# A float32 attention stage rewritten ahead of two expert stages, on one core of Trainium2

## The chip, the cores and the metric

The kernel runs on one core of one Trainium2 chip. The metric is the device time of one execution in microseconds (us). Engines are named as in the profile: PE is TensorE (its weight loads are PEld), DVE is VectorE, ACT is ScalarE, POOL is GpSimd, SP is SyncE, whose queue issues most DMAs here.

## What is computed

Three stages follow each other on 1536 tokens (2 batches of 768), all in float32.

```python
# attention: 2 x 8 heads, 768 positions, head size 64, n_sink = 4, window = 128
scores = scale * q @ k.T
keep = is_sink | ((rel >= 0) & (rel < window))
a = softmax(where(keep, scores, -1e9));  x = a @ v        # -> [1536, 512]
# SoLU block: 512 -> 1024 -> 512
h = x @ w_in;  solu = h * softmax(h);  x = (layernorm(solu) * g_ln) @ w_out
# eight dense experts, 512 -> 1024 -> 512, weighted by a Sinkhorn-normalised gate P
P = exp(x @ w_gate - max)
for _ in range(8): P /= rowsum(P); P /= colsum(P); P *= N / E
out = sum_e P[:, e] * (relu(x @ w1[e]) @ w2[e])
```

## The kernel before

Every engine has its own program, written out by hand, and semaphores between them. The engines take their instructions in order, so the order in the code is the order of the work.

**Products by splitting.** A float32 number is held as two float32r parts, `hi` (rounded) and `lo` (the rest). `three` multiplies with three matmuls (hi by hi, hi by lo, lo by hi) of 128x512, lines L495 to L497. Where a product is taken in float32 instead, the profile shows two MATMULs for one of the code.

**Attention.** The 16 heads go in eight pairs (`PAIRS`); a pair has 12 steps (`STEPS`), one head's six query tiles of 128 and then the other's. For tile t the scores are 128 x 128, 128 x 256 or, from t=2 on, 128 x 260: two blocks of keys and the four sinks.

- Loads: SP brings q and k of a head, each twice over 128 partitions, and v, and one segment of `w_in` and `w_out` beside each pair.
- Splits of q and k: POOL (`split_qk`, L324 to L335) rounds q (768 columns), subtracts on 64 partitions, rounds k and subtracts, once per head; for the first pair ACT and DVE help.
- Scores, PE L407 to L412: `q_stack` holds q's hi and lo one above the other, so two matmuls (k_hi, k_lo) make the product, and two of 4 columns the sinks. Three PSUM banks.
- `mask_max`, DVE L906: adds the mask, scales and takes the row's largest value, from PSUM to `probs` in SBUF. `exp_tile`, ACT L753: exponential and row sum.
- `invert`, DVE: L914 adds 1e-9 to six sums, L917 inverts them, L921 multiplies the sink columns. `normalise`, DVE L929: 128 x 256 from SBUF to SBUF, one instruction a tile.
- `turn`, PE L436: 22 transposes a pair of 128x128 blocks, in six groups through two banks; `turn_sinks` L443. `copy_pT`: five groups are copied from PSUM to SBUF by ACT (L759), one by DVE.
- `pv`, PE L474: float32 products of v and the turned probabilities, one head in output partitions 0 to 63 and the other in 64 to 127; `pv_sinks` L484, one product of 8 rows and 512 columns.
- `round_x` on ACT and `rest_x` on DVE (L957) split the result. `round_segments` on ACT and `rest_w_in`, `rest_w_out` on DVE (L943, L948) split the weight segments.

The pairs run in a pipeline: while pair i+1 has its scores, pair i is turned and multiplied (`body`, a hardware loop over pairs 1 to 6 on each engine).

**SoLU block.** `h1_half(T, n)` is 12 matmuls; the first four halves are set among the last pair's turns. DVE, ACT and POOL do softmax and layernorm; then transposes, `wout`, and the second split of x.

**Experts.** 16 units of half an expert. `hidden(u, g)` makes 12 groups of 12 matmuls, `expert_out(u, T)` 12 tiles of 12. POOL splits the weights: `split_unit(j)` rounds 2048 columns (L373) and subtracts (L375). Unit j=0 goes to `w_first`, j=1 to `w_unit[2:4]`, j=2 to `w_unit[0:2]`. The gate is computed by DVE between the groups of `hidden(0)`: `divide_rows` and `divide_cols` (L1125 to L1139), eight times each, with PE summing the columns by a matmul (L703) that waits for the rows. After the last one DVE copies the gate and frees PSUM banks: `y_free` starts at 2, which lets PE do two tiles of `expert_out`, and L1186 adds two.

Of the kernel before, what the change touches and what calls it, by code (L numbers as in the profile page):

```python
# [24 lines left out]
F32 = mybir.dt.float32  # L25
F32R = mybir.dt.float32r
# [33 lines left out]
def solu_moe(nc: bass.Bass, n_sink, window, qT, kT, v, w_in, w_out, g_ln, w_gate, w_exp, out):  # L60
# [5 lines left out]
    with ExitStack() as ctx:  # L66
# [34 lines left out]
        q_raw = sb("q_raw", [P, 2, SEQ], F32, in_a)  # L101
        k_raw = sb("k_raw", [P, 2, SEQ], F32, in_a)
        q_stack = sb("q_stack", [P, 2, SEQ], F32R, in_a)
        k_hi = sb("k_hi", [P, 2, SEQ], F32R, in_a)
        k_lo = sb("k_lo", [P, 2, SEQ], F32R, in_a)
        v_sb = sb("v_sb", [P, 2, QT * DH], F32, in_a)
        v_sink = sb("v_sink", [2 * NS, P], F32, in_a)
        probs = sb("probs", [P, STEPS, PW], F32, in_a)
# [4 lines left out]
        mask0 = sb("mask0", [P, P], F32, in_a)  # L113
        mask1 = sb("mask1", [P, 2 * P], F32, in_a)
        mask2 = sb("mask2", [P, PW], F32, in_a)
        a_stat = sb("a_stat", [P, 4, STEPS], F32, in_a)
# [21 lines left out]
        q_loaded = [sem(f"q_loaded{h}") for h in range(2)]  # L138
        k_loaded = [sem(f"k_loaded{h}") for h in range(2)]
        v_loaded = [sem(f"v_loaded{h}") for h in range(2)]  # L140
        vs_loaded = sem("vs_loaded")
# [9 lines left out]
        first_rounded, qk_rounded = sem("first_rounded"), sem("qk_rounded")  # L151
        q_split, k_split = sem("q_split"), sem("k_split")
        scores_full, scores_read = sem("scores_full"), sem("scores_read")
        exp_done = sem("exp_done")
        norm_link = sem("norm_link")
# [4 lines left out]
        va_used = sem("va_used")  # L160
        x_full, x_hi_out, x_out = sem("x_full"), sem("x_hi_out"), sem("x_out")
        seg_hi, seg_done = sem("seg_hi"), sem("seg_done")
# [24 lines left out]
        S_BANKS, ST_BANK, T_BANK, X_BANK = 3, 3, 4, 6  # L187
        X0 = 2 * P
# [4 lines left out]
        def p_block(h, n):  # L193

            t = (n + 1) // 2
            at = P if (n % 2 == 0 and t > 0) else 0
            return probs[:, QT * h + t, at:at + P]

        def t_group(m):

            h, g = divmod(m, 3)
            return h, 4 * g, min(4 * g + 4, NBLK)

        PT_ON_ACT = (0, 1, 3, 4, 5)
        PT_ON_DVE = (2,)
# [25 lines left out]
        def _(sp):  # L231
            def load_q(p, h):
                sp.dma_start(q_raw[:, h, :], qT[p, h]).then_inc(q_loaded[h], 16)

            def load_k(p, h):
                sp.dma_start(k_raw[:, h, :], kT[p, h]).then_inc(k_loaded[h], 16)
# [6 lines left out]
            for h in range(2):  # L243
                load_q(0, h)
                load_k(0, h)
            for h in range(2):
                sp.dma_start(v_sb[:, h, :], v[0, h]).then_inc(v_loaded[h], 16)
            sp.wait_ge(consts, 4)
            for h in range(2):
                sp.dma_start(v_sink[h * NS:(h + 1) * NS, h * DH:(h + 1) * DH],  # L250
                             v[0, h, 0:NS, 0:DH]).then_inc(vs_loaded, 16)
            sp.dma_start(g_col[:, :], g_ln).then_inc(small_loaded, 16)
            sp.dma_start(wg_raw[:, :, :], w_gate).then_inc(small_loaded, 16)
            load_segments(0)

            def load_next(i):

                for h in range(2):
                    sp.wait_ge(q_split, 2 * i + (h + 1))
                    load_q(i + 1, h)  # L260
                    sp.wait_ge(k_split, 2 * i + (h + 1))
                    load_k(i + 1, h)

            def load_beside(i):

                sp.wait_ge(seg_done, 2 * i)
                load_segments(i)
                sp.wait_ge(va_used, i)
                sp.dma_start(v_sb[:, 0, :], v[i, 0]).then_inc(v_loaded[0], 16)

            load_next(0)
            with sp.Fori(1, PAIRS - 1) as i:
                load_next(i)
                load_beside(i)
            load_beside(PAIRS - 1)

            sp.wait_ge(seg_done, 2 * FC)
# [11 lines left out]
        def _(pool):  # L289
# [30 lines left out]
            def split_qk(p, h):  # L320

                pool.wait_ge(q_loaded[h], 16 * p + 16)
                pool.sem_inc(pool_passed, 1)
                pool.tensor_scalar(q_stack[:, h, :], q_raw[:, h, :], 1.0, 0.0,  # L324
                                   ALU.mult, ALU.add).then_inc(qk_rounded, 1)
                pool.wait_ge(qk_rounded, 4 * p + (2 * h + 1 - 4))
                pool.tensor_tensor(q_stack[64:128, h, :], q_raw[64:128, h, :],
                                   q_stack[64:128, h, :].bitcast(F32), ALU.subtract).then_inc(q_split, 1)
                pool.wait_ge(q_split, 2 * p + (h + 1))
                pool.wait_ge(k_loaded[h], 16 * p + 16)  # L330
                pool.sem_inc(pool_passed, 1)
                pool.tensor_scalar(k_hi[:, h, :], k_raw[:, h, :], 1.0, 0.0,
                                   ALU.mult, ALU.add).then_inc(qk_rounded, 1)
                pool.wait_ge(qk_rounded, 4 * p + (2 * h + 2 - 4))
                pool.tensor_tensor(k_lo[:, h, :], k_raw[:, h, :], k_hi[:, h, :].bitcast(F32),  # L335
                                   ALU.subtract).then_inc(k_split, 1)


            pool.wait_ge(masks, 4)
            pool.wait_ge(q_split, 1)  # L340
            pool.wait_ge(k_split, 1)
            pool.wait_ge(first_rounded, 3)
            pool.tensor_tensor(q_stack[64:128, 1, :], q_raw[64:128, 1, :],
                               q_stack[64:128, 1, :].bitcast(F32), ALU.subtract).then_inc(q_split, 1)
            pool.wait_ge(q_split, 2)
            pool.wait_ge(first_rounded, 4)
            pool.tensor_tensor(k_lo[:, 1, :], k_raw[:, 1, :], k_hi[:, 1, :].bitcast(F32),
                               ALU.subtract).then_inc(k_split, 1)
            with pool.Fori(1, PAIRS) as p:
                for h in range(2):  # L350

                    pool.wait_ge(scores_full, STEPS * p + (QT * h - QT))
                    split_qk(p, h)


# [38 lines left out]
        def _(pe):  # L394
            def scores(p, k):

                h, t = divmod(k, QT)
                if t == 0:
                    pe.wait_ge(q_split, 2 * p + (h + 1))
                    pe.wait_ge(k_split, 2 * p + (h + 1))  # L400
                if not (isinstance(p, int) and STEPS * p + k < S_BANKS):
                    pe.wait_ge(scores_read, STEPS * p + (k - S_BANKS + 1))
                o = bank(k % S_BANKS)
                q = q_stack[:, h, t * P:(t + 1) * P]
                lo = max(t - 1, 0) * P
                hi = (t + 1) * P
                pe.matmul(o[:, 0:hi - lo], q, k_hi[:, h, lo:hi], start=True, stop=False)  # L407
                last = pe.matmul(o[:, 0:hi - lo], q, k_lo[:, h, lo:hi], start=False, stop=True)  # L408
                if t >= 2:
                    pe.matmul(o[:, 2 * P:PW], q, k_hi[:, h, 0:NS], start=False, stop=False,  # L410
                              skip_group_check=True)
                    last = pe.matmul(o[:, 2 * P:PW], q, k_lo[:, h, 0:NS], start=False, stop=True,  # L412
                                     skip_group_check=True)
                last.then_inc(scores_full, 1)

            def turn(p, m):

                h, n0, n1 = t_group(m)
                if m % 3 == 0:
                    pe.wait_ge(probs_ready, 2 * p + (h + 1))  # L420

                if m >= 2:
                    free = m - 2
                    pair = 0
                else:
                    free = m + 4
                    pair = -1
                if free in PT_ON_ACT:
                    n = len(PT_ON_ACT)
                    pe.wait_ge(pT_act, n * p + (n + n * pair + PT_ON_ACT.index(free) + 1))  # L430
                else:
                    n = len(PT_ON_DVE)
                    pe.wait_ge(pT_dve, n * p + (n + n * pair + PT_ON_DVE.index(free) + 1))
                o = bank(T_BANK + m % 2)
                for n in range(n0, n1):
                    last = pe.transpose(o[:, (n - n0) * P:(n - n0 + 1) * P], p_block(h, n), ident[:, :])  # L436
                last.then_inc(pT_full, 1)

            def turn_sinks(p):

                pe.wait_ge(sinkT_out, p + 1)
                for t in range(2, QT):
                    last = pe.transpose(bank(ST_BANK)[0:2 * NS, (t - 2) * P:(t - 1) * P],  # L443
                                        sinks[:, t - 2, :], ident[:, :])
# [784 lines left out]
```

## Time and profile before

| | |
|---|---|
| three runs | 1359.62, 1362.14, 1365.0 us; median 1362.14 |
| the profiled execution | 1365.01 us, its span 1363.2 us |
| mean granted TensorE clock | 0.984 |
| PE busy | 1322.8 us, 97% of the span |
| DVE, ACT, POOL busy | 498.5 us (37%), 259.1 (19%), 319.5 (23%) |
| DMA | 56.94 MB, mean 42 GB/s |

The busy shares are means over three very different stages: attention until about 148 us, the SoLU block until about 308 us, then the gate and the experts. Each has to be read by itself. Matmuls are pipelined and their ends modelled, so the distance from one start to the next says more than a duration.

### The profile page before, as it was taken

The numbers are of one execution on the slowest core, as the hardware profiler recorded it, in microseconds if no ns is written. First come the engines' busy times: TensorE is split into PE (matmuls) and PEld (weight loads), VectorE is DVE, ScalarE is ACT, GpSimd is POOL, SyncE is SP. The second block draws the span as 40 slices with busy tenths as digits, with TensorE's granted clock in tenths as the row PEclk, the third lists the DMA queues.
The fourth block names the chain that finished last, engine by engine and source line by source line (L and its number), as shares of the span: only waits on it lengthen the run. The fifth ranks groups of instructions, "written<-read, shape, count | busy, mean of one in ns | idle before, by whom it ended". The sixth has DMA issues, their size and how long they took to land.

```text
span 1363.2 us, 16251 instructions
## 1 busy us (share of the span) xinstructions
PE 1322.8 (97%) x6103; PEld 1088.8 (80%) x6103; DVE 498.5 (37%) x964; ACT 259.1 (19%) x555; POOL 319.5 (23%) x179
## 2 busy tenths in 40 slices
PE   5888999998999999999999999999999999999999
PEld 5666788876888888888888888888888888888887
DVE  6888553526422222222222222222222222222222
ACT  5655543421010102020101010111101010101020
POOL 6555021332011112222211111111111111111110
PEclk9888999999999999999999999999999999999999
DMA  5442200001000000000011100000000000000002
GB/s 167 147 146 95 64 0 1 1 31 62 0 31 31 31 31 31 31 31 31 31 33 44 46 31 31 31 31 31 31 31 31 31 31 31 31 31 31 31 0 93
DMA packets 15988, 56.94 MB, mean 42 GB/s; under 512 B 2144, under 2 KB 4192, under 8 KB 11872
## 3 DMA queue, kind: packets, MB, share of 16 engines
q1 hardware_dynamic: 14848, 55.28, 11.8%
q10 hardware_dynamic: 1120, 1.39, 0.3%
q8 instruction: 13, 0.21, 0.1%
q14 instruction: 7, 0.06, 0.0%
HBM read 53.51 MB, written 3.15 MB: 42 GB/s over the span
## 4 chain that ended last, share of the span: by engine, by line
PE 91%; DVE 5%; issue 2%; ACT 1%; DVEq 0%; ACTq 0%
PE ps L495 28%; PE ps L497 28%; PE ps L496 28%; PE ps L436 2%; DVE probs L929 1%; DVE probs L906 1%; PE ps L407 1%; PE ps L474 1%; PE ps L576 1%; PE ps L408 1%; PE ps L484 1%; PE ps L443 0%; DVE acc L1038 0%; ACT acc L812 0%; PE ps L412 0%
## 5 line engine op out<-in xcount | busy, mean ns | idle before, releaser
L495 PE MATMUL ps<-w_unit,h_hi 128*128 128x512 f32 x768 | 298.9, 389 | 0.0
L497 PE MATMUL ps<-w_unit,h_lo 128*128 128x512 f32 x768 | 298.8, 389 | 0.0
L496 PE MATMUL ps<-w_unit,h_hi 128*128 128x512 f32 x768 | 298.8, 389 | 0.0
L884 ACT ACTIVATE h_hi<-ps 128x512 fp32r<-128x512 f32 x192 | 114.9, 598 | 908.2 <-PE ps L497 908.2
L495 PE MATMUL ps<-x_hi,w_unit 128*128 128x512 f32 x720 | 280.1, 389 | 0.0
L496 PE MATMUL ps<-x_lo,w_unit 128*128 128x512 f32 x720 | 280.1, 389 | 0.0
L497 PE MATMUL ps<-x_hi,w_unit 128*128 128x512 f32 x720 | 280.1, 389 | 0.0
L1182 DVE SCALAR_TENSOR_TENSOR acc<-ps,gate_now,acc 128x512 f32<-128x512 f32 x192 | 144.2, 751 | 355.5 <-PE ps L497 355.5
L1107 DVE SCALAR_TENSOR_TENSOR h_lo<-ps,h_hi 128x512 fp32r<-128x512 f32 x192 | 132.7, 691 | 385.2 <-ACT h_hi L884 385.2
L373 POOL TENSOR_SCALAR w_unit<-w_raw 128x2048 fp32r<-128x2048 f32 x31 | 59.5, 1919 | 813.1 <-PE ps L497 808.0
L495 PEld LDWEIGHTS ps<-w_unit,h_hi 128*128 128x128 f32 x768 | 144.1, 188 | 30.1
L497 PEld LDWEIGHTS ps<-w_unit,h_lo 128*128 128x128 f32 x768 | 144.1, 188 | 29.9
L496 PEld LDWEIGHTS ps<-w_unit,h_hi 128*128 128x128 f32 x768 | 144.1, 188 | 29.9
L495 PEld LDWEIGHTS ps<-x_hi,w_unit 128*128 128x128 f32 x720 | 135.1, 188 | 28.2
L497 PEld LDWEIGHTS ps<-x_hi,w_unit 128*128 128x128 f32 x720 | 135.1, 188 | 28.0
L496 PEld LDWEIGHTS ps<-x_lo,w_unit 128*128 128x128 f32 x720 | 135.1, 188 | 28.0
L375 POOL TENSOR_TENSOR w_unit<-w_raw,w_unit 128x2048 fp32r<-128x2048 f32 x31 | 142.8, 4605 | 2.6
L407 PE MATMUL ps<-k_hi,q_stack 128*128 128x256 f32 (+1 forms) x96 | 42.2, 439 | 19.5 <-DVE a_stat L906 12.4
L753 ACT ACTIVATE probs<-probs,a_stat 128x260 f32<-128x260 f32 (+1 forms) x96 | 46.7, 487 | 55.2 <-DVE a_stat L906 54.9
L436 PE MATMUL ps<-ident,probs 128*128 128x128 f32 x176 | 36.4, 339 | 11.6 <-DVE probs L929 9.3
L407 PEld LDWEIGHTS ps<-k_hi,q_stack 128*128 128x128 f32 x96 | 24.2, 253 | 27.2 <-DVE a_stat L906 16.9
L929 DVE TENSOR_SCALAR probs<-probs,a_stat 128x256 f32<-128x256 f32 (+1 forms) x96 | 44.9, 484 | 0.0
(129 smaller groups left out, 1120.7 us busy)
## 6 DMA issues: line engine op xcount, KB each, us to landing
w_raw<-w_exp SPq DMA_DIRECT2D x32, 1024.0 KB, 4.8
q_raw<-qT SPq DMA_DIRECT2D x16, 384.0 KB, 4.3
k_raw<-kT SPq DMA_DIRECT2D x16, 384.0 KB, 3.9
out<-acc SPq DMA_DIRECT2D x12, 256.0 KB, 2.0
w_raw<-w_in SPq DMA_DIRECT2D x8, 256.0 KB, 2.6
w_raw<-w_out SPq DMA_DIRECT2D x8, 256.0 KB, 2.9
v_sb<-v SPq DMA_DIRECT2D x9, 192.0 KB, 2.4
v_sb<-v ACTq DMA_DIRECT2D x7, 192.0 KB, 2.9
```

Source lines behind the costliest of these rows:

```text
L373: pool.tensor_scalar(hi, w_raw[:, :], 1.0, 0.0, ALU.mult, ALU.add).then_inc(unit_rounded, 1)
L375: pool.tensor_tensor(lo, w_raw[:, :], hi.bitcast(F32), ALU.subtract).then_inc(unit_split, 1)
L407: pe.matmul(o[:, 0:hi - lo], q, k_hi[:, h, lo:hi], start=True, stop=False)
L436: last = pe.transpose(o[:, (n - n0) * P:(n - n0 + 1) * P], p_block(h, n), ident[:, :])
L495: pe.matmul(o, ws[0], xs[0], start=first, stop=False)
L496: pe.matmul(o, ws[0], xs[1], start=False, stop=False)
L497: return pe.matmul(o, ws[1], xs[0], start=False, stop=last)
L753: act.activation(probs[:, k, 0:w], probs[:, k, 0:w], ACT.Exp, bias=a_stat[:, A_NMAX, k:k + 1], scale=-1.0, accum_out=a_stat[:, A_SUM, k:k ...
L884: act.activation(h_hi[:, g, :], bank(g % 4), ACT.Relu).then_inc(h_hi_out, 1)
L929: last = dve.tensor_scalar(probs[:, k, 0:w], probs[:, k, 0:w], a_stat[:, A_INV, k:k + 1], None, ALU.mult)
L1107: dve.scalar_tensor_tensor(out=h_lo[:, g, :], in0=bank(g % 4), scalar=0.0, in1=h_hi[:, g, :].bitcast(F32), op0=ALU.max, op1=ALU.subtract). ...
L1182: dve.scalar_tensor_tensor(out=acc[:, T, :], in0=bank(4 + T % 4), scalar=gate_now[:, T:T + 1], in1=acc[:, T, :], op0=ALU.mult, op1=ALU.add ...
```

## The change

- **Scores** are float32 products, one matmul a tile, with q and k as loaded. The two heads of a pair lie on partitions 0 to 63 and 64 to 127 (`q_sb`, `k_sb`), and step t does both heads one after the other in the queue, into two of four banks. `split_qk` goes. `k_sb` holds for each tile its 256 keys and the four sinks next to them, so SP issues four DMAs a head for q and k (one with 16-byte pieces). q, k, v are double-buffered by pair.
- **Inverse sums** stay on DVE, now for four tiles at a time (three times a pair), and `normalise` moves to POOL, four tiles at a time (`BATCHES`).
- **Turns** go in three batches of both heads (3, 4 and 4 blocks), and the sinks' turn takes its place in the same two banks (`SINK_USE`), after the second use and its pair. ACT copies uses 0, 2, 4, 5, DVE copies 1, 3, 6. `turn` of batch 0 is at step t=4 of its own pair, those of batches 1 and 2 at t=0 and t=2 of the next.
- **Weight segments**: rounding and subtracting both on POOL (`round_segments`, `rest_w_in`, `rest_w_out`).
- The loops over pairs are written out.
- **Experts**: `split_unit(1)` follows `split_unit(0)` and writes the free half of `w_first`; `split_unit(2)` waits for the eighth row division (`rows_done`).

```diff
+            def load_qk(p, h):
+                rows_h = slice(64 * h, 64 * h + 64)
+                k_ph = kT[p, h][0:DH]
+                sp.dma_start(q_sb[rows_h, p % 2, :], qT[p, h][0:DH]).then_inc(qk_loaded[p % 2], 16)
...
             for h in range(2):
-                load_q(0, h)
-                load_k(0, h)
+                load_qk(0, h)
             for h in range(2):
-                sp.dma_start(v_sb[:, h, :], v[0, h]).then_inc(v_loaded[h], 16)
+                load_qk(1, h)
             sp.wait_ge(consts, 4)
             for h in range(2):
+                load_v(0, h)
+            load_segments(0)
...
+            for p in range(1, PAIRS):
+                if p >= 2:
+                    sp.wait_ge(scores_full, STEPS * (p - 1))
+                    for h in range(2):
+                        load_qk(p, h)
+                sp.wait_ge(in_done, p)
+                sp.wait_ge(out_done, p)
+                load_segments(p)
+                if p >= 2:
+                    sp.wait_ge(x_full, p - 1)
+                    for h in range(2):
+                        load_v(p, h)
...
+            def normalise(p, b):
+
+                pool.wait_ge(inv_ready, BATCHES * p + b + 1)
+                for k in range(4 * b, 4 * b + 4):
+                    w = min(k // 2 + 1, 2) * P
+                    last = pool.tensor_scalar(tile_probs(p, k)[:, 0:w], tile_probs(p, k)[:, 0:w],
+                                              a_stat[:, A_INV, k:k + 1], None, ALU.mult)
+                last.then_inc(probs_ready, 1)
...
+            round_segments(0)
+            for p in range(PAIRS):
+                normalise(p, 0)
+                rest_w_in(p)
+                normalise(p, 1)
+                rest_w_out(p)
+                normalise(p, 2)
+                if p + 1 < PAIRS:
+                    round_segments(p + 1)
...
             split_unit(0, w_first[:, 0, 0:UW], w_first[:, 1, 0:UW])
+            split_unit(1, w_first[:, 0, UW:2 * UW], w_first[:, 1, UW:2 * UW])
             pool.wait_ge(lnT_full, NB * FC)
             pool.memset(acc[:, :, :], 0.0).then_inc(acc_zero, 1)
             pool.wait_ge(o_full, o_index(NB - 1, DC - 1) + 1)
-            split_unit(1, w_unit[:, 2, :], w_unit[:, 3, :])
+            pool.wait_ge(rows_done, SINKHORN)
             split_unit(2, w_unit[:, 0, :], w_unit[:, 1, :])
...
+                for h in range(2):
+                    k = 2 * t + h
+                    n = STEPS * p + k
+                    if n >= S_BANKS:
+                        pe.wait_ge(scores_read, n - S_BANKS + 1)
+                    rows_h = slice(64 * h, 64 * h + 64)
+                    w = width(t)
+                    pe.matmul(bank(k % S_BANKS)[:, 0:w], q_sb[rows_h, p % 2, t * P:(t + 1) * P],
+                              k_sb[rows_h, p % 2, k_at(t), 0:w], start=True, stop=True).then_inc(scores_full, 1)
...
+            def back(p, t):
+
+                if t == 0 and p > 0:
+                    turn(p - 1, 1)
+                if t == 1 and p > 0:
+                    pv(p - 1, 1)
+                if t == 2 and p > 0:
+                    turn_sinks(p - 1)
+                    turn(p - 1, 2)
+                if t == 3 and p > 0:
+                    pv(p - 1, 2)
+                    pv_sinks(p - 1)
+                if t == 4:
+                    turn(p, 0)
+                if t == 5:
+                    pv(p, 0)
...
+            for p in range(PAIRS):
+                for t in range(QT):
+                    scores(p, t)
+                    back(p, t)
             h1_half(0, 0)
+            back(PAIRS, 0)
             h1_half(0, 1)
+            back(PAIRS, 1)
             h1_half(1, 0)
+            back(PAIRS, 2)
             h1_half(1, 1)
+            back(PAIRS, 3)
...
+            for p in range(PAIRS):
+                for t in range(QT):
+                    if t == 4 and p > 0:
+                        round_x(p - 1)
+                    for h in range(2):
+                        exp_tile(p, 2 * t + h)
+                    back(p, t)
```

ACT's `back` copies batch 1 of head 0 at t=0, the turned sinks and batch 2 at t=2, batch 0 at t=4. DVE's `back` is this:

```diff
+                if t == 0 and p > 0:
+                    invert(p - 1, 2)
+                    copy_pT(p - 1, 1, 1)
+                if t == 2:
+                    invert(p, 0)
+                    if p > 0:
+                        copy_pT(p - 1, 2, 1)
+                if t == 4:
+                    invert(p, 1)
+                    if p > 0:
+                        rest_x(p - 1)
+                    copy_pT(p, 0, 1)
```

## Rows read from the trace of the kernel before

**Rows 1.** Windows: busy time of each engine, granted clock, DMA share, GB/s.

```profile
core 0: us, PE busy (x) PEld busy (x) DVE busy (x) ACT busy (x) POOL busy (x), PEclk, DMA share, GB/s
29.50:137.05 107.55, 89.75 (x577) 71.40 (x577) 93.02 (x281) 64.45 (x202) 62.92 (x47) 0.83 0.38 124
30.00:34.00 4.00, 4.00 (x21) 3.65 (x22) 1.95 (x5) 2.44 (x7) 3.70 (x3) 1.00 0.02 4
148.15:166.09 17.94, 17.94 (x98) 13.11 (x99) 8.09 (x19) 6.25 (x12) 1.95 (x3) 1.00 0.21 72
...
322.00:324.00 2.00, 2.00 (x7) 1.61 (x7) 1.56 (x8) 0.00 (x0) 0.00 (x0) 0.50 0.71 147
...
345.00:1363.20 1018.20, 1014.99 (x4478) 839.93 (x4476) 285.04 (x404) 108.30 (x181) 189.32 (x58) 1.00 0.09 32
```

**Rows 2.** Groups by line and shape, DVE, 29.5 to 137.05 us: count, busy, mean.

```profile
L929 DVE TENSOR_SCALAR probs<-probs,a_stat 128x256 f32<-128x256 f32 x60 | 31.4, 524 | 0.0
L906 DVE CUSTOM_DVE_ANT_0 probs<-ps,mask 128x260 f32<-128x260 f32 x49 | 20.3, 414 | 0.9 <-PE ps L412 0.8
L921 DVE TENSOR_TENSOR sinks<-probs,a_stat 128x16 f32<-128x16 f32 x12 | 13.7, 1138 | 0.4
L914 DVE TENSOR_SCALAR a_stat<-a_stat 128x6 f32<-128x6 f32 x12 | 9.5, 792 | 0.1
...
L957 DVE TENSOR_TENSOR x_lo<-ps,x_hi 128x512 f32 x5 | 3.4, 675 | 0.0
```

**Rows 3.** Order of time, DVE and POOL: start, duration, instruction.

```profile
68.46 0.17 DVE L914 TENSOR_SCALAR a_stat<-a_stat 128x6 f32<-128x6 f32 x1
...
77.28 0.83 POOL L332 TENSOR_SCALAR k_hi<-k_raw 128x768 fp32r<-128x768 f32 x1 [0.22 <-POOL q_stack L327]
...
78.05 2.10 DVE L929 TENSOR_SCALAR probs<-probs,a_stat 128x128 f32<-128x128 f32 x2
...
78.19 1.81 POOL L335 TENSOR_TENSOR k_lo<-k_raw,k_hi 128x768 fp32r<-128x768 f32 x1
```

**Rows 4.** The chain of waits, one piece: start, duration, instructions.

```profile
29.50 1.11 PE ps L436 x4
```

**Rows 5.** Order of time, PE, 72 to 79 us.

```profile
72.33 1.08 PE L474 MATMUL ps<-pT,v_sb 128*64 128x256 f32 x8 [0.36 <-ACT pT L759]
...
76.59 1.12 PE L484 MATMUL ps<-sinkT,v_sink 8*128 8x512 f32 x2
77.64 0.66 PE L436 MATMUL ps<-ident,probs 128*128 128x128 f32 x4
78.05 0.36 PE L407 MATMUL ps<-k_hi,q_stack 128*128 128x256 f32 x1
...
78.51 0.36 PE L407 MATMUL ps<-k_hi,q_stack 128*128 128x256 f32 x1
```

**Rows 6.** Order of time in the gate: POOL, DVE, PE.

```profile
316.99 4.49 POOL L375 TENSOR_TENSOR w_unit<-w_raw,w_unit 128x2048 fp32r<-128x2048 f32 x1
...
317.23 4.37 DVE L1128 TENSOR_TENSOR gate<-gate,rows 128x96 f32<-128x96 f32 x1
...
321.66 0.74 PE L703 MATMUL ps<-gate,ones 128*128 128x96 f32 x2 [4.51 <-DVE gate L1128]
```

**Rows 7.** Groups by line and shape, ACT, 0 to 210 us.

```profile
L753 ACT ACTIVATE probs<-probs,a_stat 128x260 f32<-128x260 f32 x64 | 32.2, 504 | 5.9 <-DVE a_stat L906 5.7
```

**Rows 8.** Order of time at the start: SP's queue and PE.

```profile
5.71 0.43 SPq L241 DMA_DIRECT2D w_raw<-w_out  x1
...
7.11 0.45 PE L407 MATMUL ps<-k_hi,q_stack 128*128 128x128 f32 x1 [7.11 <-DVE k_lo L975]
```

**Rows 9.** The page's DMA issues: count, KB, us from issue to landing.

```profile
w_raw<-w_out SPq DMA_DIRECT2D x8, 256.0 KB, 2.9
```

**Rows 10.** Order of time at the gate's end: DVE and PE.

```profile
347.11 0.26 DVE L1128 TENSOR_TENSOR gate<-gate,rows 128x96 f32<-128x96 f32 x1
...
347.84 0.49 PE L495 MATMUL ps<-w_unit,h_hi 128*128 128x512 f32 x1
...
350.33 0.17 DVE L1186 COPY rows<-rows 128x12 f32<-128x12 f32 x1
```

More of the change, by code:

```diff
@@ L339, in _ @@
[L339 to L348, printed above, removed]
@@ L394, in _, with scores @@
         def _(pe):
-            def scores(p, k):
-                h, t = divmod(k, QT)
+            def scores(p, t):
                 if t == 0:
[L399 to L436, printed above, removed]
-                last.then_inc(pT_full, 1)
@@ new lines, in bank_free, with turn @@
+            def bank_free(p, use):
+                before = T_USES * p + use - 2
+                if before >= 0:
+                    done, n = copied(*divmod(before, T_USES))
+                    pe.wait_ge(done, n)
+            def turn(p, b):
+                pe.wait_ge(probs_ready, BATCHES * p + b + 1)
+                for h in range(2):
+                    use = t_use(b, h)
+                    bank_free(p, use)
+                    for n in range(T_FIRST[b], T_END[b]):
+                        at = (n - T_FIRST[b]) * P
+                        last = pe.transpose(t_bank(p, use)[:, at:at + P], p_block(p, h, n), ident[:, :])
+                    last.then_inc(pT_full, 1)
@@ L723, in _ @@
                               stop=True).then_inc(top_all, 1)
-            with pe.Fori(0, UNITS - 1) as u:
+            second = (w_unit[:, 2, :], w_unit[:, 3, :])
+            for T in range(NT):
+                expert_out(0, T, (w_first[:, 0, UW:2 * UW], w_first[:, 1, UW:2 * UW]))
+            for g in range(GROUPS):
+                hidden(1, g, (w_unit[:, 0, :], w_unit[:, 1, :]))
+            with pe.Fori(1, UNITS - 1) as u:
                 for T in range(NT):
-                    expert_out(u, T)
+                    expert_out(u, T, second)
                 for g in range(GROUPS):
@@ L788, in _ @@
-            act.activation(wg[:, :, 0:EXPERTS], wg_raw[:, :, :], ACT.Copy).then_inc(wg_ready, 1)
-            def body(i, before):
-                for k in range(STEPS):
-                    back(i, k)
-                    exp_tile(i + 1, k)
-                    if k == 2 and before:
-                        round_x(i - 1)
-                        load_v(i, 1)
-                        load_sinks(i)
-                    if k == QT - 1:
-                        round_segments(i)
-            body(0, False)
@@ L803, in _, with back @@
-            with act.Fori(1, PAIRS - 1) as i:
-                body(i, True)
+                act.activation(x_hi[:, p * SEQ:(p + 1) * SEQ], x_psum(0, QT), ACT.Copy).then_inc(x_hi_out, 1)
+            def back(p, t):
+                if t == 0 and p > 0:
+                    copy_pT(p - 1, 1, 0)
+                if t == 2 and p > 0:
+                    copy_sinkT(p - 1)
+                    copy_pT(p - 1, 2, 0)
+                if t == 4:
+                    copy_pT(p, 0, 0)
+            for p in range(PAIRS):
+                for t in range(QT):
+                    if t == 4 and p > 0:
+                        round_x(p - 1)
+                    for h in range(2):
+                        exp_tile(p, 2 * t + h)
+                    back(p, t)
+                if p == 0:
+                    act.wait_ge(small_loaded, 32)
+                    act.activation(wg[:, :, 0:EXPERTS], wg_raw[:, :, :], ACT.Copy).then_inc(wg_ready, 1)
@@ L993, in behind @@
-            def behind(p, k):
-                if k < QT:
-                    spread(p, 1, k)
-            for k in range(STEPS):
-                front(0, k)
-            dve.wait_ge(wg_ready, 1)
-            dve.tensor_tensor(wg[:, :, EXPERTS:2 * EXPERTS], wg_raw[:, :, :],
-                              wg[:, :, 0:EXPERTS].bitcast(F32), ALU.subtract).then_inc(wg_ready, 1)
-            def body(i, before):
-                for k in range(STEPS):
-                    back(i, k)
-                    front(i + 1, k)
-                    behind(i, k)
-                    if k == QT - 1 and before:
-                        rest_x(i - 1)
-                    if k == QT + 1:
-                        rest_w_in(i)
-                    if k == QT + 2:
-                        rest_w_out(i)
@@ L1016, in _ @@
-            body(0, False)
-            with dve.Fori(1, PAIRS - 1) as i:
-                body(i, True)
-            rest_w_in(PAIRS - 1)
-            for k in range(QT):
-                behind(PAIRS - 1, k)
-            rest_w_out(PAIRS - 1)
-            rest_x(PAIRS - 2)
-            copy_pT(PAIRS - 1, 2)
+                s = slice(p * SEQ, (p + 1) * SEQ)
+                dve.tensor_tensor(x_lo[:, s], x_psum(0, QT), x_hi[:, s].bitcast(F32),
+                                  ALU.subtract).then_inc(x_out, 1)
@@ new lines, in _ @@
+            dve.wait_ge(masks, 4)
+            for p in range(PAIRS):
+                for t in range(QT):
+                    for h in range(2):
+                        mask_max(p, 2 * t + h)
+                    back(p, t)
+                if p == 0:
+                    dve.wait_ge(wg_ready, 1)
+                    dve.tensor_tensor(wg[:, :, EXPERTS:2 * EXPERTS], wg_raw[:, :, :],
+                                      wg[:, :, 0:EXPERTS].bitcast(F32), ALU.subtract).then_inc(wg_ready, 1)
+            invert(PAIRS - 1, 2)
```

416 lines of the change are left out of this document (143 added, 273 removed).

## The prediction

> **What bounds the kernel now.** Read the windows first [rows 1]. The first row runs from one pair's first transposes to those six pairs later: 107.55 us, so 17.9 us a pair, and there are eight pairs. Divided by six, DVE is busy 15.5 us in each, PE 15.0, ACT 10.7, POOL 10.5. The last row starts after the gate: PE is busy 1014.99 of 1018.20 us, so expert blocks go at PE's pace and nothing in this change speeds them. All that can move lies ahead of 345 us. There PE is the bound from 148.15 us on, where the first `h1_half` starts and the window is cut: 17.94 busy of 17.94. One hole in the gate excepted, that lasts. Before 148.15 us DVE is the bound, though not by arithmetic alone. The DVE groups [rows 2] show what it does: normalising, `mask_max`, inverse sums. The inverse's 128x6 TENSOR_SCALAR averages 792 ns and the 16-wide `sinks` product 1138 ns. The order of time explains it [rows 3]: the first took 0.17 us at 68.46, but two normalisings started at 78.05 took 2.10 us, ending (80.15) just after POOL's k_lo subtraction (78.19 to 80.00). A DVE instruction from SBUF to SBUF stands until POOL's ends.
>
> PE is slow rather than idle. The granted clock of the six pairs is 0.83, a mean of the two levels, 1.2 and 2.4 GHz: a third of the time at the lower [rows 1]. In the chain four transposes last 1.11 us at 29.50 [rows 4], in the order of time 0.66 at 77.64 [rows 5]; so PE ran at the lower pace at first too, though the column reads 1.00 there.
>
> **The change, per pair.** DVE loses ten normalisings of 524 ns and two narrower ones [rows 2], the two weight subtractions (675 ns class, like L957's [rows 2]), and the long stands. It keeps twelve masks at 0.35 us from one start to the next (4.2 in all, estimate from 414 ns with its overlap) and rest_x, 0.95 us for 768 columns (675 ns for 512). It gains two copies of pT (0.6 us for 512 columns, by L957): 1.7 for three. Inverses come three times: 0.2+0.2+0.2 us when nothing stands in the way, so 1.7; by the means in [rows 2] (792 and 1138 ns) they would be 5.3. I take 2.0: POOL is idle at two of the three. DVE: 4.2+0.95+1.7+2.0 = 8.9 us. It stops being the bound.
>
> POOL loses all q/k splitting and gains normalising and weight splits. By 0.83 us for 768 columns [rows 3] and a slope of 0.84 ns a column (its subtraction of 2048 columns takes 4.49 us [rows 6], one of 768 takes 1.81 [rows 3]: 2.1 ns a column, and rounding goes at 0.4 of that) a TENSOR_SCALAR costs 0.40 us for 256, 0.62 for 512, and a subtraction of 512 is 1.25. So 4.6 + 1.2 + 2.5 = 8.3 us.
>
> ACT loses the weight roundings (1.2 us) and one copy: twelve exponentials at 0.5 us a step (504 ns [rows 7]), four copies at 0.5 (by the same), round_x 0.8: 8.7 us.
>
> PE. A float32 product is two instructions at two cycles a column: the sink product, two of 512 columns, 1.12 us [rows 5] and 1.05 until the next starts, 0.85 of it columns. The eight pT instructions of 256 columns took 1.08 us. One after another they would need 1.71, so two heads in separate column halves run side by side. Scores before: four instructions a tile, 78.05 to the next tile's at 78.51, 0.45 us, 5.3 a pair. After: 1424 columns a head at four cycles, 2.4 us if heads overlap in row halves, 4.7 if not. I take overlap with 0.1 us a step on top, by what these products take beyond their columns: 3.0. Transposes 22 x 0.11 = 2.4 (four from 77.64 to 78.05 [rows 5]), the sinks' 0.45, pT products of 384, 384 and 640 columns a head 0.80+0.80+1.23, sink product 1.05. PE: 9.7 us at 2.4 GHz, before about 12.
>
> The Trainium skill (TensorEngine Tiling (Array Packing), Tiling Modes) says tiles of different rows work in parallel, and by it scores would be 2.4 us. The same section says that a change of tiling mode drains the array, which speaks against this change, as row-tiled scores now alternate with whole-array transposes and column-tiled products. No row here shows a row-tiled product. The column-tiled ones leave room for a drain of about 0.2 us [rows 5].
>
> No engine is full, so the period is a chain. From the end of the masks of step t=4 to the same point of the next pair, at 2.4 GHz: inverse 0.65, rest_x 0.95, copy 0.5, masks 0.75 and 0.5 (3.35); ACT's last exponentials of the pair end at 3.6; inverse 0.65, copy 0.6 (4.85); PE product 0.80 and scores 0.5, hand-over 0.2, masks 0.75 (7.1); ACT exponential 0.7 and `copy_sinkT` 0.5 (8.3), for which the second half of `turn(p-1, 2)` waits, since its bank held sinkT, and behind it in PE's queue the scores of t=3; transposes 0.45, DVE copy 0.7 (9.5); products 1.23 and 1.05, scores 0.5, hand-over 0.2, masks 0.75: 13.2 us. PE's part is 4.5; a third of it at half the clock adds 1.5. Period: **14.7 us**. The normalisings hide: POOL needs 1.6 us after an inverse, while DVE does rest_x, copy and masks. If that cover went, each would put 1.6 on the chain.
>
> Loads: SP issues 14 DMAs a pair, 0.43 us each [rows 8], 6 us of 14.7. Segments reissued after `rest_w_out` (3.5 in the chain's time) land 2.9 us later [rows 9], rounding ends at 8.4, and `normalise(p, 0)` is wanted at about 12: hidden, 2 us to spare.
>
> Start: eight loads issued from 0.75 us on land by about 7 us, like the first score of before (7.11 [rows 8]). But the first segments come 21st and 22nd in SP's queue: issued by 10.6, landed by 14.2, rounded by 15.4, and only then is `normalise(0, 0)` done (16.8). PE stands at `turn(0, 0)` with the scores of t=5 behind it; pair 0's masks end at 19.6. In the first pair before, splitting cost about as much. `h1_half` starts at 19.6 + 7 x 14.7 = 122.5 us, against 148.15: **25.6 us gained**. What PE still has to do of attention then falls from 7.0 us (17.94 [rows 1] less 48 matmuls at 0.227, which is 1014.99 over 4478) to 0.87+0.80+0.45+0.87+1.23+1.05 = 5.3: **1.7 gained**. Removing the loops' branches I price between nothing and 1 us a pair and take nothing: where code is straight the waits stay.
>
> Gate: DVE's L1128 took 4.37 us because POOL's split of unit 2 ran 316.99 to 321.48; PE waited 4.51 us [rows 6] and then ran at 1.2 GHz: granted clock 0.50 from 322 to 324 [rows 1]. Two microseconds at half pace and a little beyond lose 1.3. With unit 1 split earlier and unit 2 behind the eighth row sum, 5.8 us go. Given back: the eighth row sum ends at 347.37 [rows 10]; POOL then rounds to 349.4 and subtracts to 354.0, right across `divide_cols(7)`. By the same pattern as at 317.23 DVE's L1139 stands until 354.1 and y_free comes at 354.7 instead of 350.5. PE, in `expert_out` from 347.84, has banks for two tiles, 5.5 us, until 353.3: a wait of 1.4. **Net 4.4 gained.** Split 1 at 281 to 288, with the memset behind it, meets DVE instructions that read PSUM; I price it at nothing. If they stood too, up to 4.6 us would be PE's loss.
>
> Sum: 1363.2 - 25.6 - 1.7 - 4.4 = 1331.5 us span. The profiled execution took 1365.01, 1.8 over its span, and lies 2.9 over the median 1362.14: forecast **1330 us**.
>
> **Rivals.** (a) Scores not side by side, or the array emptied at each change of mode. Two of the chain's score steps grow by 0.45, more at half clock, with 0.5 for changes: period 16 to 17.5 us, 1339 to 1350. For it: no row-tiled product in the trace, and changes of mode in every step. (Its second half is the drain that the Trainium skill names under Tiling Modes, above.) Against: column halves do overlap. (b) The clock stays at 2.4 GHz, as in the window from 148.15 [rows 1]: period 12.4 to 13.2, 1314 to 1320. For it: less waiting. Against: the chain leaves PE idle 1.4 to 2 us at a time. (c) Slower: PE at 1.2 GHz throughout and scores serial. PE then needs (9.7 + 2.3) x 2 = 24.0 us a pair, time 1330 + 7 x 9.3 = 1395. It decides from a period of 19.2 us on, where the gain is gone. Against: from 30 to 34 us PE was busy 4.00 of 4.00 us [rows 1] at the lower pace, and by 77.64 the pace had risen [rows 5]. (d) The change moves DVE's work onto a new wait (late loads with their 16-byte pieces, or normalisings standing between DVE's instructions): period 18 to 19, 1353 to 1360, hardly a change.
>
> **From this the numbers.** Forecast 0.55 (its own range 1321 to 1340), (a) 0.19, (b) 0.15, (c) 0.05, (d) 0.06. Over 0.5% (6.8 us, about what a measurement of this kernel tells from no change) means under 1355.3 or over 1369. Forecast, (a) and (b) are faster with a little of (a)'s tail off: 0.89; same 0.06; slower 0.05. The range runs from (b)'s 1314 to 1351, just over (a)'s 1350.
>
> **What would show it.** Period of the windows near 14.7; DVE busy 9 to 10 us of it, POOL 8; PE's waits ahead of L474 and the transposes, released by ACT's sinkT copy; scores pairs starting together; first `h1_half` near 122.5 us; no 4.5 us hole in the gate, but one of 1.4 after the second `expert_out`. A period over 17, or half clock throughout, makes this wrong.

## The result and the profile after

The changed kernel took 1349.15 us (median of four runs, 1348.37 to 1349.79), the kernel before 1363.46 beside it; the ratio is 0.9896, 95% interval 0.9876 to 0.9915. So it is faster, by 1.0%, clear of the noise. The forecast was 1330 us, a gain of 2.4%. The profiled execution has a span of 1347.1 us where 1331.5 were forecast: 15.6 us are missing from the gain.

The windows show where. The first row is six pairs again, cut where `scores(p, 4)` of one pair begins and that of the sixth after it [rows 1]; then two single pairs, and the four stretches behind attention. The number after the five counts is the granted clock, 1.00 for 2.4 GHz.

```profile
36.23:131.94 95.71, 71.28 (x483) 41.73 (x482) 55.83 (x216) 55.01 (x174) 82.75 (x97) 0.96 0.46 114
...
51.77:67.29 15.52, 11.44 (x82) 6.63 (x82) 9.16 (x36) 9.20 (x29) 13.84 (x17) 1.00 0.49 125
...
99.61:116.41 16.80, 12.74 (x83) 7.46 (x82) 9.59 (x36) 9.11 (x29) 13.87 (x16) 0.90 0.51 124
...
136.28:153.47 17.19, 16.95 (x92) 12.29 (x91) 6.40 (x12) 5.49 (x11) 8.30 (x10) 1.00 0.19 62
153.47:296.96 143.49, 142.88 (x676) 116.62 (x676) 60.73 (x108) 49.45 (x82) 39.50 (x38) 1.00 0.04 15
296.96:330.10 33.14, 32.38 (x151) 25.85 (x151) 20.90 (x75) 6.46 (x12) 0.27 (x1) 1.00 0.00 1
330.10:1347.10 1017.00, 1012.28 (x4465) 837.50 (x4464) 287.20 (x395) 108.32 (x181) 195.47 (x60) 1.00 0.09 33
```

A pair takes 15.95 us on average, 15.53 at full clock and 16.80 in the two of six with clock 0.90. DVE is busy 9.3 us of it, as forecast; ACT 9.2. But POOL (the fifth number with a count) is busy 13.8 us where 8.3 were expected. The groups of POOL, 35 to 113 us, say with what:

```profile
L344 POOL TENSOR_SCALAR probs<-probs,a_stat 128x256 f32<-128x256 f32 x49 | 44.4, 922 | 9.6 <-DVE sinks L868 9.0
L368 POOL TENSOR_TENSOR w_unit<-w_raw,w_unit 128x512 fp32r<-128x512 f32 x5 | 6.4, 1275 | 0.0
...
L354 POOL TENSOR_SCALAR w_first<-w_raw 128x512 fp32r<-128x512 f32 x5 | 3.1, 616 | 0.0
```

The subtraction (1275 ns) and the rounding (616 ns) cost what was forecast, 1.25 and 0.62 us. A normalising of 256 columns costs 922 ns, more than a rounding of 512, where 400 were forecast. In the order of time of one pair (start, duration, instruction, idle time before it and its releaser) PE is seen to wait for it twice, 1.04 us before the turn at 57.65 (its weight load shows 1.23) and 0.98 before the one at 62.64:

```profile
53.98 3.62 POOL L344 TENSOR_SCALAR probs<-probs,a_stat 128x256 f32<-128x256 f32 x4 [1.55 <-DVE sinks L868]
...
57.56 1.27 POOL L368 TENSOR_TENSOR w_unit<-w_raw,w_unit 128x512 fp32r<-128x512 f32 x1
57.65 0.85 PEld L450 LDWEIGHTS ps<-ident,probs 128*128 128x128 f32 x8 [1.23 <-POOL probs L344]
...
57.86 1.00 DVE L868 TENSOR_TENSOR sinks<-probs,a_stat 128x16 f32<-128x16 f32 x1
58.96 3.62 POOL L344 TENSOR_SCALAR probs<-probs,a_stat 128x256 f32<-128x256 f32 x4
...
62.64 1.43 PE L450 MATMUL ps<-ident,probs 128*128 128x128 f32 x8 [0.98 <-POOL probs L344]
```

The second wait has a history. POOL works without a gap: 3.62 us for four normalisings, 1.27 for `rest_w_out`, 3.62 for the next four. DVE's sinks product at 57.86 stood behind `rest_w_out` for 1.00 us (0.18 when free), so the inverse for the next four came late as well, but that delayed them by only 0.1 us, since POOL itself was busy until 58.83. DVE's copy of pT at 58.79, for which PE waits, comes behind the same product.

The chain that ended last shows what of this costs time. At full clock it goes through DVE's stand, in the two pairs at the lower clock through the four normalisings themselves:

```profile
57.86 1.00 DVE sinks L868
58.86 0.62 DVE pT L877
59.62 0.87 PE ps L474 x8
...
101.82 3.63 POOL probs L344 x4
```

PE's second wait, at 62.64, is not on the chain: the other half of that turn stands in any case until 63.41, behind ACT's exponentials and `copy_sinkT`.

The start, in the order of time: PE's first scores, the release of POOL by the first weight segment, the first turn, and DVE's last mask of pair 0.

```profile
7.23 0.61 SPq L255 DMA_DIRECT2D k_sb<-kT  x1
...
8.75 4.80 PE L432 MATMUL ps<-k_sb,q_sb 64*128 64x128 f32 x20 [8.75 <-DMA k_sb<-kT]
...
16.63 0.62 POOL L354 TENSOR_SCALAR w_first<-w_raw 128x512 fp32r<-128x512 f32 x1 [11.16 <-DMA w_raw<-w_in]
...
17.89 3.00 POOL L344 TENSOR_SCALAR probs<-probs,a_stat 128x128 f32<-128x128 f32 x4
...
20.94 1.54 PE L450 MATMUL ps<-ident,probs 128*128 128x128 f32 x6 [7.39 <-POOL probs L344]
...
24.19 0.42 DVE L850 CUSTOM_DVE_ANT_0 probs<-ps,mask 128x260 f32<-128x260 f32 x1
```

An issue of q or k takes SP 0.61 us here; the forecast had 0.43, from a weight segment's [rows 8]. PE stood 7.39 us before the first turn, and pair 0's masks ended at 24.6 us instead of 19.6.

The gate came out as foreseen. No hole of 4.51 us [rows 6] is left; DVE stands once, behind POOL's split of unit 2, and PE waits 1.47 us for it:

```profile
331.83 4.58 POOL L400 TENSOR_TENSOR w_unit<-w_raw,w_unit 128x2048 fp32r<-128x2048 f32 x1
...
332.05 4.48 DVE L1030 TENSOR_TENSOR gate<-gate,cols 128x96 f32<-128x96 f32 x1
...
337.14 0.50 PE L502 MATMUL ps<-w_first,h_hi 128*128 128x512 f32 x1 [1.47 <-DVE rows L1077]
```

### The profile page after: what moved, and what is told of

It is laid out like the page before. It is cut to its first block, busy times and chain, and to the rows that moved or that the text cites. A ratio compares the mean times of both kernels' runs of the same rounds, so it can differ in the third digit from the quotient of the medians.

```text
span 1347.1 us, 15303 instructions
## 1 busy us (share of the span) xinstructions
PE 1297.1 (96%) x5975; PEld 1047.4 (78%) x5975; DVE 445.6 (33%) x874; ACT 241.2 (18%) x511; POOL 352.4 (26%) x249
## 4 chain that ended last, share of the span: by engine, by line
PE 90%; DVE 4%; ACT 2%; issue 1%; POOL 1%; SPq 1%; DMA 0%; DVEq 0%
PE ps L502 28%; PE ps L504 28%; PE ps L503 28%; PE ps L474 2%; PE ps L432 1%; PE ps L450 1%; DVE pT L877 1%; PE ps L550 1%; POOL probs L344 1%; PE ps L480 1%; ACT probs L718 1%; DVE sinks L868 0%; DVE acc L928 0%; DVE probs L850 0%; DVE gate L1030 0%
## 5 line engine op out<-in xcount | busy, mean ns | idle before, releaser
L502 PE MATMUL ps<-w_unit,h_hi 128*128 128x512 f32 x720 | 280.1, 389 | 0.0
L503 PE MATMUL ps<-w_unit,h_hi 128*128 128x512 f32 x720 | 280.1, 389 | 0.0
L504 PE MATMUL ps<-w_unit,h_lo 128*128 128x512 f32 x720 | 280.1, 389 | 0.0
L504 PEld LDWEIGHTS ps<-w_unit,h_lo 128*128 128x128 f32 x720 | 135.1, 188 | 28.1
L502 PEld LDWEIGHTS ps<-w_unit,h_hi 128*128 128x128 f32 x720 | 135.1, 188 | 28.1
L503 PEld LDWEIGHTS ps<-w_unit,h_hi 128*128 128x128 f32 x720 | 135.1, 188 | 28.0
L400 POOL TENSOR_TENSOR w_unit<-w_raw,w_unit 128x2048 fp32r<-128x2048 f32 x30 | 138.2, 4608 | 2.5
L344 POOL TENSOR_SCALAR probs<-probs,a_stat 128x256 f32<-128x256 f32 (+1 forms) x96 | 81.8, 869 | 15.1 <-DVE sinks L868 13.5
L718 ACT ACTIVATE probs<-probs,a_stat 128x260 f32<-128x260 f32 (+2 forms) x96 | 46.5, 484 | 49.4 <-DVE a_stat L850 49.3
L450 PE MATMUL ps<-ident,probs 128*128 128x128 f32 x176 | 28.7, 302 | 22.0 <-POOL probs L344 18.2
L850 DVE CUSTOM_DVE_ANT_0 probs<-ps,mask 128x260 f32<-128x260 f32 (+2 forms) x96 | 35.1, 402 | 42.5 <-PE ps L432 41.3
L450 PEld LDWEIGHTS ps<-ident,probs 128*128 128x128 f32 x176 | 21.0, 152 | 30.0 <-POOL probs L344 21.7
```

Of the source, the lines that this page charges most:

```text
L344: last = pool.tensor_scalar(tile_probs(p, k)[:, 0:w], tile_probs(p, k)[:, 0:w], a_stat[:, A_INV, k:k + 1], None, ALU.mult)
L400: pool.tensor_tensor(lo, w_raw[:, :], hi.bitcast(F32), ALU.subtract).then_inc(unit_split, 1)
L450: last = pe.transpose(t_bank(p, use)[:, at:at + P], p_block(p, h, n), ident[:, :])
L502: pe.matmul(o, ws[0], xs[0], start=first, stop=False)
L503: pe.matmul(o, ws[0], xs[1], start=False, stop=False)
L504: return pe.matmul(o, ws[1], xs[0], start=False, stop=last)
```

## The experiments

**Another form of the same instruction.** POOL's other instructions keep to their price, so the form is suspect: L344 has one operation, all its other TENSOR_SCALARs two.

```diff
-                                              a_stat[:, A_INV, k:k + 1], None, ALU.mult)
+                                              a_stat[:, A_INV, k:k + 1], 0.0, ALU.mult, ALU.add)
```

> One edit to the changed kernel: POOL's normalising multiplies by the inverse and adds 0.0 (two operations) where it had one operation and no second. Theory A (the form of the instruction is what is dear: with one operation and a scalar per partition 922 ns for 256 columns, while two-operation forms, L391 with 1024 columns in 1.2 us and L354 with 512 in 0.62, go at 0.84 ns a column): 0.40 us each, POOL 8 us a pair in place of 13.8, period from 15.9 to about 13.5 us, normalise(0, 0) 1.6 us sooner; time about 1331 us. Theory B (POOL is slow on 256 columns of these rows whatever the form, or waits for DVE's port): L344 stays at 0.9 us and the time at 1349.

1339.64 us (1337.22 to 1342.8); ratio to before 0.982, interval 0.9803 to 0.9838. POOL's row for 256 columns, 35 to 113 us, and the chain over one pair of this kernel:

```profile
L344 POOL TENSOR_SCALAR probs<-probs,a_stat 128x256 f32<-128x256 f32 x57 | 26.3, 479 | 28.9 <-DVE sinks L868 28.9
```

```profile
60.11 1.30 PE ps L474 x12
61.41 1.05 PE ps L480 x2
62.46 0.69 PE ps L432 x4
...
66.00 0.87 PE ps L474 x8
...
70.13 0.69 PE ps L432 x4
...
71.43 1.10 ACT probs L718 x4
72.53 0.48 ACT sinkT L730
73.06 0.67 PE ps L450 x4
...
74.59 1.30 PE ps L474 x12
```

Theory A holds: 479 ns, and POOL is gone from the chain. The period is 14.48 us (60.11 to 74.59), not the 13.5 of the expectation. What is left is the chain of the prediction, its items larger: four score matmuls 0.69 (forecast 0.5), ACT's exponentials 1.10 (0.7), half a turn 0.67 (0.45), the product of batch 0 (at t=5, 66.00) 0.87, which I had beside DVE's work and which lies on the chain. From that product to the next it is 3.26 us (66.00 to 69.26), in the changed kernel 4.31 (55.31 to 59.62): these 1.05 us are the whole difference of the two periods at full clock, 15.53 and 14.48.

**The price by itself.** Eleven forms, twice each with a wait between, on free memory behind POOL's last split; the rest of the kernel is unchanged (one run, 1350.7 us).

```diff
+            for _ in range(2):
+                pool.tensor_scalar(dst[:, 0:256], src[:, 0:256], ca, None, ALU.mult).then_inc(scr, 1)
+                pool.wait_ge(scr, 3 + _)
...
+            for _ in range(2):
+                pool.tensor_scalar(dst[:, 0:256], src[:, 0:256], ca, 0.0, ALU.mult, ALU.add).then_inc(scr, 1)
+                pool.wait_ge(scr, 13 + _)
```

> The changed kernel with eleven forms of POOL's TENSOR_SCALAR, twice each, on free memory at its end (no part of the result; PE is still at the last unit). Theory A (one operation with no second is what costs): 256 columns take about 0.9 us in every form with a single operation, be the factor a number or a pointer, and 0.4 to 0.5 in every form with two; 1024 columns 2.8 to 2.9 us against 1.2. Theory A' (the pointer costs, and the second operation happens to pick another routine): the single operation with a constant 1.0 is fast as well. Theory B (in-place work or the start at column 260): only those two forms are slow.

In the order of time, two instructions a row. Lines 426 to 435 have one operation with a pointer (in place at 432, from column 260 at 435), 438 one operation with a constant, 441 to 453 two operations with one or two pointers (447, 450 and 453 not shown: 0.53, 0.60 and 1.25 us each), 456 two with constants:

```profile
1289.26 1.95 POOL L426 TENSOR_SCALAR w_raw<-w_raw,stat 128x256 f32<-128x256 f32 x2
1291.30 5.78 POOL L429 TENSOR_SCALAR w_raw<-w_raw,stat 128x1024 f32<-128x1024 f32 x2
1297.17 1.94 POOL L432 TENSOR_SCALAR w_raw<-w_raw,stat 128x256 f32<-128x256 f32 x2
1299.21 1.94 POOL L435 TENSOR_SCALAR w_raw<-w_raw,stat 128x256 f32<-128x256 f32 x2
...
1301.24 1.79 POOL L438 TENSOR_SCALAR w_raw<-w_raw 128x256 f32<-128x256 f32 x2
1303.13 1.06 POOL L441 TENSOR_SCALAR w_raw<-w_raw,stat 128x256 f32<-128x256 f32 x2
1304.28 2.35 POOL L444 TENSOR_SCALAR w_raw<-w_raw,stat 128x1024 f32<-128x1024 f32 x2
...
1311.78 0.90 POOL L456 TENSOR_SCALAR w_raw<-w_raw 128x256 f32<-128x256 f32 x2
```

One operation costs 0.97 us for 256 columns and 2.9 for 1024 with a pointer, 0.9 for 256 with a constant. Two operations cost 0.53, 1.18 and 0.45. The pointer adds some 0.08 us; place and start add nothing. So the form alone sets the price, without a second operation 2.5 ns a column against 0.84 with one. Why the form without one is slower no run shows.

**Normalising back on DVE.** POOL keeps the weight splits, and in `normalise` its wait for the inverse; only the multiplications move, to DVE's `invert`.

```diff
+                for k in range(4 * b, 4 * b + 4):
+                    w = min(k // 2 + 1, 2) * P
+                    last = dve.tensor_scalar(tile_probs(p, k)[:, 0:w], tile_probs(p, k)[:, 0:w],
+                                             a_stat[:, A_INV, k:k + 1], None, ALU.mult)
+                last.then_inc(probs_ready, 1)
```

> One part of the change undone: DVE normalises (12 instructions of 0.27 us from start to start, 3.2 us a pair), POOL keeps the weight splits. Theory A (POOL's normalising, 3.6 us after each inverse, stands on the chain; DVE has 6 us a pair free): period 14 to 14.5 us, time 1336 to 1340. Theory B (POOL's time is hidden, the chain of copies and products sets the period, DVE's extra 3.2 us lie on it): period 16 or over, 1350 to 1360.

1375.13 us, ratio to before 1.0076 (1.006 to 1.0091): slower than both. Neither number was right, Theory B's direction was. The chain of this kernel over part of a pair:

```profile
96.12 0.60 DVE probs L869 x2
96.72 0.86 DVE x_lo L883
97.59 0.48 DVE pT L877
...
100.67 1.75 DVE probs L869 x4
102.42 0.61 DVE pT L877
...
106.09 2.06 DVE probs L869 x4
108.15 0.61 DVE pT L877
...
108.89 1.30 PE ps L469 x12
```

From the same product one pair earlier (90.20) to 108.89 it is 18.69 us, 4.2 more than with two operations on POOL. The granted clock was 0.91 in this stretch (1.00 in the pair of `two_op`), yet PE's pieces on the chain last as long as there, 1.30 us for twelve, so the 4.2 are not clock. Ahead of each copy of pT, for which PE waits, now stand the normalisings of a batch, with POOL's splits in their way: the 128-column ones average 808 ns in this trace against 275 before. That collision is in part made by the edit. POOL still waits for each inverse before it goes on to a split, so the split starts just when DVE starts to normalise (POOL at 100.76 and 106.08, DVE at 100.67 and 106.09). The three batches take 2.1, 1.75 and 2.06 us, where the expectation had 3.2 for all; by that estimate some 2.7 of the 4.2 us are the collision. So DVE's idle 6 us a pair were not at the places where this work went, and normalising on DVE in this form is slower than on POOL even in the dear form. A version whose splits do not wait for the inverse, or with the normalisings at another place in DVE's order, was not run, and it might do as well as the changed kernel.

**Order of SP's queue.**

```diff
             for h in range(2):
                 load_qk(0, h)
+            load_segments(0)
+            sp.wait_ge(consts, 4)
+            for h in range(2):
+                load_v(0, h)
             for h in range(2):
                 load_qk(1, h)
-            sp.wait_ge(consts, 4)
-            for h in range(2):
-                load_v(0, h)
-            load_segments(0)
```

> One edit to the changed kernel: SP issues the first weight segments and v of pair 0 ahead of pair 1's q and k. Theory A (the first normalising waits for the 22nd DMA in SP's queue): the segments land about 5 us sooner (13.0 - 5.9 = 7 us of issuing less, but they then share the DMA engines with pair 0's keys), pair 0 ends 4 to 5 us sooner, time 1344.5. Theory B (v, or the loads of pair 1 that come later, take over as what pair 0 or 1 waits for): 1347 to 1349.

1345.18 us, ratio to before 0.9852 (0.9837 to 0.9867), 4 us under the changed kernel; the first turn starts at 15.65 us instead of 20.94. Theory A, with a part of the 5.3 us lost again on the way: the first `h1_half` comes 3.3 us sooner (132.95), and this run had three stretches of lower clock in attention (0.77, 0.89 and 0.89 in windows of 15 us; the changed kernel had two pairs at 0.90).

**The expert part alone**, on the kernel before: unit 1 split early, unit 2 behind the eighth row sum. PE reads unit 1 where it now lies (its part of the edit is not shown).

```diff
             split_unit(0, w_first[:, 0, 0:UW], w_first[:, 1, 0:UW])
+            split_unit(1, w_first[:, 0, UW:2 * UW], w_first[:, 1, UW:2 * UW])
...
-            split_unit(1, w_unit[:, 2, :], w_unit[:, 3, :])
+            pool.wait_ge(rows_done, SINKHORN)
             split_unit(2, w_unit[:, 0, :], w_unit[:, 1, :])
```

> The expert part of the change alone on the kernel before: unit 1 split after unit 0 into w_first, unit 2 behind the eighth row sum. From the traces: the hole of 4.51 us and 1.2 us of half clock go, 1.47 us are given back; net 4.2 us, ratio 0.997. Rival: the split of unit 1 lies in the SoLU block and disturbs DVE there: net under 2 us.

1360.59 us (1359.72 to 1361.25), ratio to before 0.9964 (0.9952 to 0.9976), the span 3.8 us shorter (1359.4). PE's only long wait in the gate is the 1.5 us for DVE. The early split of unit 1 costs nothing that shows: from the first `h1_half` to the gate's first transposes it is 160.84 us with it and without. By difference the attention part of the change is worth 0.7%.

**The sinks' copy off the chain**, on top of the two-operation form.

```diff
                 if t == 1 and p > 0:
+                    turn_sinks(p - 1)
                     pv(p - 1, 1)
                 if t == 2 and p > 0:
-                    turn_sinks(p - 1)
                     turn(p - 1, 2)
...
+                if t == 1 and p > 0:
+                    copy_sinkT(p - 1)
                 if t == 2 and p > 0:
-                    copy_sinkT(p - 1)
                     copy_pT(p - 1, 2, 0)
```

> Two edits to the changed kernel: the two-operation normalising, and the sinks turned by PE at t=1 and copied by ACT right after (before: at t=2, behind that step's exponentials). Theory A (the step of the prediction's chain in which the second half of the turn waits for ACT's sinkT copy, 1.3 to 1.6 us a pair in the trace of the two-operation kernel): period 14.5 to about 13.2 us, 7 to 9 us under that kernel's 1339.6: 1331. Theory B (the wait moves: DVE's and ACT's copies of the same step, or PE's own queue of products, take its place): 1337 to 1340.

1330.66 us (1330.08 to 1331.09), ratio to before 0.9747 (0.9732 to 0.9762). The period is 13.53 us (chain: `pv` of twelve instructions at 58.10, 71.63 and 85.17), 0.95 less, and the clock column reads 1.00 throughout. The wait that the prediction named was real. Seven periods make 6.7 us of the 9.0 between the medians; `two_op` had runs at a lower clock, `sink_early` hardly any.

**Together.** `combo` has the two-operation form, SP's order and this:

```diff
-            pool.wait_ge(rows_done, SINKHORN)
+            pool.wait_ge(gate_col, 1)
```

> Three edits to the changed kernel: two-operation normalising, first segments and v issued ahead of pair 1's loads, and POOL's split of unit 2 behind DVE's first gate column rather than the eighth row sum. If the costs are separate they add up: 1339.6 - 3.4 to 5 (start) - 1.5 (the wait of expert_out's third tile): 1333 to 1335. If the early segments only mattered while normalising was slow: 1338.

1338.26 us (1335.14 to 1339.49), ratio 0.9797 (0.9782 to 0.9812): 3 to 5 us worse than the sum. The number of the second guess, 1338, was met, but not its reason: the 1.5 us wait in the gate is gone, and the first turn is 5.1 us ahead of that of `two_op` (14.18 against 19.27). Then the first `h1_half` comes 4.0 us later than there (128.74 against 124.72), since TensorE's clock dropped in four of eight windows:

```profile
45.00:60.00 15.00, 11.68 (x70) 6.56 (x70) 6.92 (x30) 8.20 (x27) 9.01 (x16) 0.85 0.57 133
60.00:75.00 15.00, 13.18 (x74) 8.30 (x74) 8.39 (x36) 7.71 (x27) 8.97 (x16) 0.70 0.56 133
...
105.00:120.00 15.00, 13.93 (x64) 7.60 (x60) 6.82 (x31) 6.95 (x24) 6.46 (x13) 0.61 0.27 74
```

With all four edits the clock stays:

> All four edits together. Sum of the separate ones: 1326 if the sink edit is worth 8 us, 1334 if it is worth nothing. Faster than the changed kernel (1349) either way, by 1.1 to 1.7%.

1323.4 us (1323.17 to 1323.75), ratio to before 0.9696 (0.9683 to 0.9709); 1.9% under the changed kernel by the medians and 2.6 us under the lower of the two sums. Granted clock 1.00 in every window, first `h1_half` at 112.94 us against 136.28.

## Why the prediction was wrong in size

**What bounds it**: right. Experts go at PE's pace before and after (1014.99 of 1018.20 us [rows 1], 1012.28 of 1017.00 now).

**DVE, ACT, PE per pair**: right within 0.5 us for two, DVE 9.3 us for 8.9, ACT 9.2 for 8.7. PE is busy 11.4 us for 9.7 by counted work, 1.7 more. The heads' scores run side by side: four instructions of 260 columns take 0.69 us in the chain, while one after another they would need 1.07 at the pace of the sinks' product (1024 columns in 1.05 us). So the first half of rival (a) did not come. Side by side their columns alone would take 0.43 us, by an estimate from the prediction's two cycles a column. What they take over that leaves room for the drain at a change of mode of which the Trainium skill speaks (TensorEngine Tiling (Array Packing), Tiling Modes), but no run separates it.

**POOL**: this step failed, in the sentence that a TENSOR_SCALAR costs 0.40 us for 256 columns, and with it "The normalisings hide". I took the slope of instructions with two operations for one with a single operation. It costs 0.92. Even with two operations it costs 0.48 in this place, 0.08 of it for the pointer. Four of them, 3.6 us, do not fit under DVE's rest_x, copy and masks; the stand of DVE behind `rest_w_out` follows from them. PE waits for them twice a pair, but only the first wait is on the chain. The price that I named for lost cover was 1.6 us for each; paid were 1.05 us a pair at full clock, once. Two-operation normalising brings back 11.7 us of the 15.6 missing (spans 1347.1 and 1335.4), 9.5 by the medians. That is shown. Up to the first `h1_half` its 11.6 us add up: 1.7 at the first turn, seven times 1.05, and twice 1.26 for the two pairs that ran at the lower clock.

**The chain and its clock term**: two errors that offset. At full clock the chain with cheap normalising is 14.48 us, not 13.2 (scores, exponentials and turn too small, one product misplaced). The clock term was 1.5 us and came out at 0.4 (15.95 against 15.53), in `two_op` at nothing from 35 us on. Together they gave 14.7, so the close agreement with 14.48 is luck. The period of the changed kernel is 14.48 + 1.05 for the normalisings + 0.42 for the clock, 15.95.

**Start**: the place was right, the size not: 24.6 us instead of 19.6. Issues of 0.61 us put the first scores at 8.75 and the segments at 16.6; normalising took 3.0 us instead of 1.4; the first turn ran at the lower clock by its pace, 1.54 us for six instructions against 1.09 for eight at 57.65 (the clock column reads 1.00 at both). Of the 5.0 us that is 2.4, 1.6 and about 1.0.

**The sum**: start +5.0; seven periods of 15.93 instead of 14.7, +8.6; +0.2 to the first `h1_half` (136.28 against 122.5). Then 1210.8 us to the end against 1209.0: PE's rest of attention 6.3 us (17.19 less 10.9) against 5.3, the SoLU block 0.6 longer, gate 4.1 gained against 4.4 (38.85 to 33.14 before `expert_out`, 1.64 given back behind it).

**Gate**: right, in mechanism and size.

**Rivals**: the measured time lies at the end of (a)'s times, but for another reason, as said above. (b), full clock throughout, did not come in the changed kernel (0.96 over six pairs); it came in `sink_early` and `best`, at a period of 13.5. (d) named normalisings standing in DVE's way; what happened is near it, DVE behind POOL's split once a pair, at a period of 15.9 rather than 18. (c) is refuted: the clock was at 2.4 GHz most of the time.

## What to carry to other kernels

Price an instruction that moves to another engine by a row of that engine in the same form, the number of operations included; if none is in the trace, keep both ends apart until one is measured. Cover is a matter of place: DVE had 6 us idle a pair, and 3 us of normalising put among its other work made the pair 18.69 us long, against 15.95 with the dear form on POOL. When work moves off an engine, the waits that it needed should go with it: those left on POOL set its splits against DVE. And a shorter wait on PE can pay twice, where the clock then holds: from `combo` to `best` the sinks' copy gave 1.1%, at granted clock 1.00 in place of 0.61 to 0.94 in four windows.

## What the hardware showed that was not expected

- POOL's TENSOR_SCALAR with one operation: 0.97 us for 128x256 and 2.9 for 128x1024 float32; with an added `+ 0.0`: 0.53 and 1.18.
- SP issued each of the first loads of q and k, over 64 partitions, in 0.57 to 0.62 us, where loads over 128 partitions took 0.43 [rows 8]. But the number of partitions is not shown to be the cause: in `combo` the segment of `w_in`, over 128 partitions, took 0.61 right behind them, and the next q 0.49 behind v.
- Small changes of timing decide whether TensorE's clock falls in attention: it read 1.00 throughout with `sink_early` and `best` and 0.61 to 0.94 in four windows of `combo`. It also differs from one run of a kernel to the next: `two_op` had mean clocks from 0.991 to 1.000 and spans from 1341.0 to 1336.1 us (1335.4 at 0.997). What tips it was not settled.
